# Second expert by Strassen's seven products in 924-token rounds, with combined split weights prepared by GpSimd beside the first expert

## The chip, the cores and the metric

The kernel runs on one core of one Trainium2 chip. The metric is the device time of one execution in microseconds (us), lower is better. TensorE (PE) multiplies matrices, VectorE (DVE) and ScalarE (ACT) do elementwise work and can read PSUM, GpSimd (POOL) does elementwise work on SBUF only, SyncE (SP) issues most of the DMAs. Each engine works through its own list in order and waits on semaphores.

## The reference

Three stages run one after the other on 4608 tokens (8 batches of 576), in float32:

```
p_packed = sm_attn(p, k, v)              # 32 packed keys per head
out      = sm_attn(q, p_packed, p_packed)
x        = out as (4608, 512)
xn = x / rms(x) * rms_g                  # first expert, d_ff 1536
x  = (silu(xn @ w_gate) * (xn @ w_val)) @ w_out
h  = x @ w_in                            # second expert, d_ff 2048
g  = max(h, 0) + alpha * min(h, 0)
y  = g @ w_out2
```

## The kernel before

Every large product is made from split operands: a float32 value is cast to a rounded part `hi` (float32r) and the remainder `lo`, and `three_passes` (lines 736 to 740) multiplies w_hi by hi, w_lo by hi and w_hi by lo into one PSUM bank. So each tile product is three matmuls, and each activation tile needs a cast (ScalarE) and a subtraction (VectorE) before it can be used.

The first part of the program (about 0 to 737 us) joins attention and first expert. It runs by batch. Tile b of the first expert is 24 half blocks: SiLU on ScalarE (line 1305), the product with `val` on VectorE (line 1655), the cast of h to `h_hi` (line 1313), the subtraction for `h_lo` (line 1659), and the products of two blocks earlier. Between the half blocks stands the attention of the next batch, placed by tables (`PE_PLACES`, `LATER` and the like), and the folding of the packed values into the gate and val weights (`m_hi`, `m_lo`, line 934), which reads `gv_sb`, all 12 chunks of the gate and val weights, held in SBUF. GpSimd only scales `pp_t` (line 655) and normalises `a2` (line 660) there. SyncE issues the DMAs in program order: for each half block pair the last 64 tokens of the batch go to `rest_mid` (line 531), and ScalarE waits for that store before it reuses the slot of `act_sb`. From batch 7 on SyncE also loads the second expert's weights, and GpSimd splits them (lines 711 and 713). A last tile of the gathered 8 x 64 tokens closes the first expert.

The second expert (737 us to the end) runs over nine tiles of 512 tokens. All its split weights lie in SBUF (`w2_hi_*`, `w2_lo_*`). GpSimd splits each tile's input (lines 718 and 720, four chunks of 512 columns), two tiles deep. Per tile there are 16 hidden blocks: 4 products up, 4 products down, three blocks behind. VectorE makes the leaky ReLU in two instructions (lines 1692 and 1695), ScalarE casts (line 1346), VectorE subtracts (line 1699). The down products accumulate over all 16 blocks in four PSUM banks, which ScalarE copies out (line 1355) and stores.

## Time and profile before

| | us |
|---|---|
| median of 3 runs | 1525.37 (1524.71 to 1525.61) |
| span of the profiled execution | 1524.0 |
| second expert, from its first matmul to the end of the span | 737.1 to 1524.0 |
| PE busy | 1513.6 |
| DVE busy | 726.7 |
| ACT busy | 444.7 |
| POOL busy | 193.0 |

The profiled execution's own time is known by its span alone, 1524.0 us from first to last instruction. Matmuls are pipelined, so a row's duration is longer than the distance to the next matmul: it is the distance between starts that fills the time. An instruction's recorded time contains what it waits for after it has started.

### The profile page before, as it was taken

How to read it: one execution, taken by the hardware profiler on the slowest of the kernel's cores; microseconds unless marked ns; L12 is line 12 of the kernel's file. 1: busy time of each engine (PE TensorE's matmuls, PEld its weight loads, DVE VectorE, ACT ScalarE, POOL GpSimd, SP SyncE). 2: the span in 40 equal slices, each digit the busy share in tenths (PEclk: the TensorE clock that was granted, in tenths of full speed). 3: DMA queues.
4: the chain of work that ended last, by engine and by line, in shares of the span. 5: the costliest groups of instructions: out<-in, count | busy, mean ns of one | idle time of the engine just before them, and what ended most of it. 6: DMA issues, size and time to landing. Idle time of an engine off the chain costs nothing.

```text
span 1524.0 us, 23354 instructions
## 1 busy us (share of the span) xinstructions
PE 1513.6 (99%) x9430; PEld 1258.5 (83%) x9430; DVE 726.7 (48%) x1234; ACT 444.7 (29%) x789; POOL 193.0 (13%) x197
## 2 busy tenths in 40 slices
PE   8999999999999999999999999999999999999999
PEld 5988888888888888898888888888888888888887
DVE  6674756555564746543443333333333333333333
ACT  4554544534544544422111111111111111111111
POOL 2700000000000000263342020020202001020000
PEclk9999999999999999999999999999999999999999
DMA  9313232130313230242301000010100000010000
GB/s 359 114 42 100 67 99 68 66 101 33 103 36 99 67 98 6 75 136 107 138 1 55 0 28 28 10 47 0 56 0 35 22 28 28 0 55 1 28 0 28
DMA packets 62080, 90.16 MB, mean 59 GB/s; under 512 B 17056, under 2 KB 32416, under 8 KB 61600
## 3 DMA queue, kind: packets, MB, share of 16 engines
q1 hardware_dynamic: 56944, 79.78, 16.5%
q10 hardware_dynamic: 5040, 8.98, 1.5%
q8 instruction: 75, 1.23, 0.3%
q14 instruction: 21, 0.17, 0.0%
HBM read 63.19 MB, written 25.56 MB: 58 GB/s over the span
## 4 chain that ended last, share of the span: by engine, by line
PE 98%; DVE 1%; ACT 0%; DMA 0%; issue 0%; SPq 0%; POOL 0%; POOLq 0%; DVEq 0%
PE psum L738 31%; PE psum L740 30%; PE psum L739 30%; PE psum L934 3%; PE psum L761 1%; PE psum L837 1%; PE psum L810 1%; PE psum L1074 0%; PE psum L866 0%; PE psum L865 0%; PE psum L869 0%; DMA a_keys<-a_mid 0%; PE psum L795 0%; SPq L515 0%; DMA a_mid<-a_rows 0%
## 5 line engine op out<-in xcount | busy, mean ns | idle before, releaser
L1699 DVE TENSOR_TENSOR h_lo<-g,h_hi 128x512 fp32r<-128x512 f32 x144 | 106.5, 739 | 470.2 <-ACT h_hi L1346 470.2
L1346 ACT CAST h_hi<-g 128x512 fp32r<-128x512 f32 x144 | 89.4, 621 | 632.7 <-PE psum L740 599.8
L738 PE MATMUL psum<-an_hi,m_hi 128*128 128x288 f32 x768 | 232.1, 302 | 1.2 <-DVE an_lo L1554 1.2
L740 PE MATMUL psum<-an_lo,m_hi 128*128 128x288 f32 x768 | 225.8, 294 | 0.0
L739 PE MATMUL psum<-an_hi,m_lo 128*128 128x288 f32 x768 | 225.8, 294 | 0.0
L738 PE MATMUL psum<-h_hi,ow_hi 128*128 128x512 f32 (+2 forms) x480 | 182.8, 381 | 0.0
L740 PE MATMUL psum<-h_lo,ow_hi 128*128 128x512 f32 (+2 forms) x480 | 177.7, 370 | 0.0
L739 PE MATMUL psum<-h_hi,ow_lo 128*128 128x512 f32 (+2 forms) x480 | 177.4, 370 | 0.0
L738 PEld LDWEIGHTS psum<-an_hi,m_hi 128*128 128x128 f32 x768 | 144.0, 188 | 24.1 <-issue 14.8
L1655 DVE TENSOR_TENSOR act_sb<-act_sb,psum 128x288 f32<-128x288 f32 x168 | 75.7, 451 | 154.2 <-PE psum L740 136.5
L739 PEld LDWEIGHTS psum<-an_hi,m_lo 128*128 128x128 f32 x768 | 144.3, 188 | 4.2
L740 PEld LDWEIGHTS psum<-an_lo,m_hi 128*128 128x128 f32 x768 | 144.2, 188 | 0.0
L738 PE MATMUL psum<-h_hi,w_hi_front 128*128 128x512 f32 x360 | 140.1, 389 | 0.0
L740 PE MATMUL psum<-h_lo,w_hi_front 128*128 128x512 f32 x360 | 140.1, 389 | 0.0
L740 PE MATMUL psum<-xs,w_hi_front 128*128 128x512 f32 x360 | 140.0, 389 | 0.0
L738 PE MATMUL psum<-xs,w_hi_front 128*128 128x512 f32 x360 | 140.0, 389 | 0.0
L739 PE MATMUL psum<-xs,w_lo_front 128*128 128x512 f32 x360 | 140.0, 389 | 0.0
L739 PE MATMUL psum<-h_hi,w_lo_front 128*128 128x512 f32 x360 | 140.0, 389 | 0.0
L1305 ACT ACTIVATE act_sb<-psum 128x288 f32<-128x288 f32 x168 | 69.0, 411 | 200.7 <-PE psum L740 200.1
L738 PEld LDWEIGHTS psum<-h_hi,ow_hi 128*128 128x128 f32 x480 | 90.2, 188 | 38.2 <-issue 27.3
L1692 DVE TENSOR_SCALAR act_sb<-psum,alpha_sb 128x512 f32<-128x512 f32 x144 | 107.4, 746 | 2.0 <-PE psum L740 2.0
L740 PEld LDWEIGHTS psum<-h_lo,ow_hi 128*128 128x128 f32 x480 | 90.3, 188 | 16.3
(183 smaller groups left out, 2405.6 us busy)
## 6 DMA issues: line engine op xcount, KB each, us to landing
k_sb<-k_t SPq DMA_DIRECT2D x16, 576.0 KB, 5.2
q_sb<-q_t SPq DMA_DIRECT2D x8, 1152.0 KB, 5.5
xs_raw<-y_mid SPq DMA_DIRECT2D x9, 1024.0 KB, 5.2
out_t<-o_sb ACTq DMA_DIRECT2D x34, 256.0 KB, 2.0
gv_sb<-w_gv SPq DMA_DIRECT2D x6, 1024.0 KB, 17.1
...
a_keys<-a_mid SPq DMA_DIRECT2D x24, 160.0 KB, 3.3
```

The costliest lines, as they stand in the source:

```text
L738: nc.tensor.matmul(dst, w_hi, hi, start=start, stop=False)
L739: nc.tensor.matmul(dst, w_lo, hi, start=False, stop=False)
L740: return nc.tensor.matmul(dst, w_hi, lo, start=False, stop=stop)
L761: mm = nc.tensor.matmul(dst, p_sb[dims, pair, :], k_sb[dims, pair, h * HALF:(h + 1) * HALF], start=True, stop=True)
L810: mm = nc.tensor.matmul(pp_ps(c, e)[PACK * pair:PACK * (pair + 1), :], a_keys[:, e * PAIRS + pair, j, :], v_sb[:, j, head * HEAD_DIM:(head ...
L837: mm = nc.tensor.matmul(s2_ps(e)[PACK * pair:PACK * (pair + 1), :], pp_t[dims, pair, :], q[dims, pair, h * HALF:(h + 1) * HALF], start=Tru ...
L934: mm = nc.tensor.matmul(psum[keys, m_bank(c, j) + e, :].rearrange("p (f n) -> p f n", f=2), pp_tg[dims, pair, :], gv_sb[dims, 2 * j:2 * j ...
L1305: nc.scalar.activation(act_sb[:, s, half * HALF:(half + 1) * HALF], gate_ps, ACT.Silu).then_inc(silu_done, 1)
L1346: nc.scalar.copy(h2_hi[:, f % 2, :], g32[:, f % 2, :]).then_inc(g_hi_done, 1)
L1655: nc.vector.tensor_tensor(dst, dst, val_ps, ALU.mult).then_inc(h32_done, 1)
L1692: nc.vector.tensor_scalar(act2_sb[:, s, :], h, 0.0, alpha_sb[:, f:f + 1], ALU.min, ALU.mult).then_inc(neg_done, 1)
L1699: nc.vector.tensor_tensor(h2_lo[:, s, :], g32[:, s, :], h2_hi[:, s, :].bitcast(F32), ALU.subtract).then_inc(g_lo_done, 1)
```

## The change

The second expert is computed by Strassen's scheme in Winograd's form. Both its products are cut into two by two blocks: for the up product two halves of the 512 model dimensions, two neighbouring hidden blocks (a duo, 8 of them), and two halves of a round's tokens; for the down product the same with the roles exchanged. Instead of eight block products there are seven, of sums and differences of blocks. A round has 924 tokens (2 x 462; the last 2 x 456), and there are five rounds. The matmuls are 462 columns wide.

- Weights: GpSimd (`combine`) makes from each of 32 parts of raw weights four combinations, casts the seven matrices to hi and subtracts for lo. This stands in the first expert's tiles 1 to 7, up to two parts before `scaled` and three behind it. SyncE stores hi and lo to DRAM (`w_up`, `w_down`), in runs of 512 bytes, and later streams them back page by page (30 pages a round, of 786 KB or 1 MB) into a ring of four slots.
- To make room, the first expert holds only 6 chunks of `gv_sb` and loads each pair of chunks again in every batch (33 loads of 1 MB).
- Input: GpSimd makes four differences of 2 x 462 columns and splits seven matrices of 2 x 462 columns a round, as soon as the previous round's up products are done; two sums of outputs stand between the fourth and the fifth split.
- Up: 42 matmuls a duo. VectorE and ScalarE evict seven PSUM results (three of them accumulate onto an evicted bank), ScalarE makes the two halves of the leaky ReLU, VectorE joins them.
- Down: 56 units a round, each one staged block times two output halves, 6 matmuls. ScalarE casts the block to `stage_hi`, VectorE subtracts for `stage_lo`; four stages. VectorE makes the differences of blocks (`difference`) and sums of outputs (`down_sums`) in between, by a table of places (`BESIDE_UNITS`). All down products of a round follow all its up products.

The instruction counts in the second expert: 3456 matmuls of 512 columns before, 5 x 672 = 3360 of 462 (456) now.

```diff
+PRODUCTS = 7
...
+PART_PLACES = {b: ([5 * (b - 1), 5 * (b - 1) + 1], [5 * (b - 1) + n for n in range(2, 5)]) for b in range(1, BATCH)}
...
+WIDTHS = [462, 462, 462, 462, 456]
...
+UNIT_SLOTS, STAGES = 4, 4
...
+    w_up = nc.dram_tensor("w_up", (DUOS, P, PRODUCTS, 2, 2, P), F32, kind="Internal").ap()
+    w_down = nc.dram_tensor("w_down", (PRODUCTS, P, DUOS, 2, 2, P), F32, kind="Internal").ap()
...
+            def load_part(n):
+                slot = n % PART_SLOTS
+                reached(sp, part_out[slot], 32 * (n // PART_SLOTS))
+                raw = parts_raw[slot]
+                sp.dma_start(raw[:, 0:PRODUCTS:3, :], w2_parts[n, :, 0:3, :]).then_inc(part_in[slot], 16)
+                sp.dma_start(raw[:, 4, :], w2_parts[n, :, 3, :]).then_inc(part_in[slot], 16)
+
+            def store_part(n):
+                sp.wait_ge(part_ready, n + 1)
+                slot, j, side = n % PART_SLOTS, n % (2 * DUOS) // 2, n % 2
+                for level, src in ((0, parts_hi[slot]), (1, parts_lo[slot])):
+                    if n < 2 * DUOS:
+                        dst = w_up[j, :, :, side, level, :]
+                    else:
+                        dst = w_down[:, :, j, side, level, :].rearrange("i p n -> p i n")
+                    sp.dma_start(dst, src[:].bitcast(F32)).then_inc(part_out[slot], 16)
...
+            def move_parts(b, f):
...
+                    for n in range(PART_SLOTS):
+                        load_part(n)
+                if f == 3:
+                    for n in early:
+                        store_part(n)
+                if f == 4:
+                    for n in early:
+                        if n + PART_SLOTS < PARTS:
+                            load_part(n + PART_SLOTS)
...
+            def load_x(t):
+                w, at = WIDTHS[t], STARTS[t]
+                for slot, rows, cols in ((0, 0, 0), (2, 0, 1), (4, 2, 0), (5, 2, 1)):
+                    sp.dma_start(x_raw[:, slot, :, 0:w],
+                                 y_mid[:, rows:rows + 2, at + cols * w:at + (cols + 1) * w]).then_inc(x_in, 16)
...
+            def load_page(t, n):
+                q, slot = PAGES * t + n, (PAGES * t + n) % UNIT_SLOTS
...
+                if q >= UNIT_SLOTS:
+                    free_t, free_n = (q - UNIT_SLOTS) // PAGES, (q - UNIT_SLOTS) % PAGES
+                    if free_n < 2 * DUOS:
+                        sp.wait_ge(up_mm, PRODUCTS * (DUOS * free_t + free_n // 2) + UP_PARTS[free_n % 2][1])
+                    else:
+                        sp.wait_ge(unit_mm, UNITS * free_t + DUOS * (free_n // 2 - DUOS) + DOWN_PARTS[free_n % 2][1])
+                sp.dma_start(ring[:, slot, 0:stop - first_unit].bitcast(F32), src).then_inc(ring_in[slot], 16)
+
...
+            def combine(n):
...
+                nc.gpsimd.tensor_tensor(raw[:, 2, :], raw[:, 3, :], raw[:, 6, :], ALU.add).then_inc(part_step, 1)
+                pool.wait_ge(part_step, done + 1)
+                nc.gpsimd.tensor_tensor(raw[:, 3, :], raw[:, 0, :], raw[:, 3, :], ALU.subtract).then_inc(part_step, 1)
+                nc.gpsimd.tensor_tensor(raw[:, 1, :], raw[:, 2, :], raw[:, 0, :], ALU.subtract).then_inc(part_step, 1)
+                pool.wait_ge(part_step, done + 3)
+                nc.gpsimd.tensor_tensor(raw[:, 5, :], raw[:, 4, :], raw[:, 1, :], ALU.subtract).then_inc(part_step, 1)
+                pool.wait_ge(part_step, done + 4)
+                nc.gpsimd.tensor_copy(hi[:], raw[:]).then_inc(part_step, 1)
+                pool.wait_ge(part_step, done + 5)
+                nc.gpsimd.tensor_tensor(lo[:], raw[:], hi[:].bitcast(F32), ALU.subtract).then_inc(part_ready, 1)
...
+                early, late = PART_PLACES.get(c - 1, ([], []))
+                for n in early:
+                    combine(n)
+                if c < BATCH:
+                    scaled(c)
+                for n in late:
+                    combine(n)
+                if c < BATCH:
+                    normed(c, 0)
+                    normed(c, 1)
...
+            def differences(t):
+                w, done = WIDTHS[t], X_STEPS * t
+                pool.wait_ge(x_in, 16 * 4 * (t + 1))
+                for n, (to, of, less) in enumerate(((3, 5, 2), (2, 2, 0), (1, 5, 2), (6, 4, 1))):
+                    nc.gpsimd.tensor_tensor(x_raw[:, to, :, 0:w], x_raw[:, of, :, 0:w], x_raw[:, less, :, 0:w],
+                                            ALU.subtract).then_inc(x_step, 1)
+                    pool.wait_ge(x_step, done + n + 1)
+
+            def split_x(t, i):
+                w, done = WIDTHS[t], X_STEPS * t + 4 + i
+                nc.gpsimd.tensor_copy(x_hi[:, i, :, 0:w], x_raw[:, i, :, 0:w]).then_inc(x_step, 1)
+                pool.wait_ge(x_step, done + 1)
+                nc.gpsimd.tensor_tensor(x_lo[:, i, :, 0:w], x_raw[:, i, :, 0:w], x_hi[:, i, :, 0:w].bitcast(F32),
+                                        ALU.subtract).then_inc(x_ready, 1)
...
+            def sums_of_outs(t):
...
+                nc.gpsimd.tensor_tensor(out_f[:, :, 0:w], out_e[:, :, 0:w], out_h[:, :, 0:w], ALU.add).then_inc(f_done, 1)
+                pool.wait_ge(f_done, t + 1)
+                nc.gpsimd.tensor_tensor(out_h[:, :, 0:w], out_r[:, :, 0:w], out_h[:, :, 0:w], ALU.add).then_inc(q_done, 1)
...
+            differences(0)
+            for i in range(PRODUCTS):
+                split_x(0, i)
+            for t in range(ROUNDS):
+                if t + 1 < ROUNDS:
+                    differences(t + 1)
+                    for i in range(4):
+                        split_x(t + 1, i)
+                sums_of_outs(t)
+                if t + 1 < ROUNDS:
+                    for i in range(4, PRODUCTS):
...
+            def up(t, j):
+
+                w, n = WIDTHS[t], DUOS * t + j
+                freed = {0: (c11_copied, n), 1: (u_done, n), 2: (c12_done, n), 3: (c21_done, n),
+                         4: (p1_copied, n + 1), 5: (c22_part, n + 1), 6: (c22_done, n + 1)}
+                for part, (begin, end) in enumerate(UP_PARTS):
...
+                    for i in range(begin, end):
...
+                        dst = four_ps(UP_BANKS[i], w)
+                        for k in range(2):
+                            mm = three_passes(dst, weights[:, i - begin, k, 0, :], weights[:, i - begin, k, 1, :],
+                                              x_hi[:, i, k, 0:w], x_lo[:, i, k, 0:w], k == 0 and i < 4, k == 1, i >= 4)
...
+            def down2(t, p):
...
+                        u = UNITS * t + DUOS * p + j
+                        pe.wait_ge(stage_lo_done, u + 1)
+                        for side in range(2):
...
+            def stage_hi_of(t, u):
+                w, p, j, n = WIDTHS[t], u // DUOS, u % DUOS, UNITS * t + u
+                i = DOWN_ORDER[p]
...
+                reached(act, unit_mm, n - STAGES + 1)
+                nc.scalar.copy(stage_hi[:, n % STAGES, 0:w], raw_of(i, j, w)).then_inc(stage_hi_done, 1)
...
+            def negative(t, j, f):
...
+                nc.scalar.activation(below[:, f, :, 0:w], g_sb2[:, j, f, :, 0:w], ACT.Relu, scale=-1.0).then_inc(below_done, 1)
...
+            def up_sums(t, j, name):
+                w, n = WIDTHS[t], DUOS * t + j
+                u, c22 = shared[:, n % 2, 0:w], g_sb2[:, j, 1, 1, 0:w]
+                if name == "u":
+                    dve.wait_ge(up_mm, PRODUCTS * n + 2)
+                    dve.wait_ge(p1_copied, n + 1)
+                    nc.vector.tensor_tensor(u, first_p[:, 0:w], four_ps(1, w), ALU.add).then_inc(u_done, 1)
...
+            def joined(t, j, f):
+                w, n = WIDTHS[t], DUOS * t + j
+                dve.wait_ge(above_done, 2 * n + f + 1)
+                both = g_sb2[:, j, f, :, 0:w]
+                nc.vector.scalar_tensor_tensor(out=both, in0=below[:, f, :, 0:w], scalar=minus_alpha[:, 2 * j + f:2 * j + f + 1],
+                                               in1=both, op0=ALU.mult, op1=ALU.add).then_inc(g_done, 1)
...
+            def stage_lo_of(t, u):
+                w, p, j, n = WIDTHS[t], u // DUOS, u % DUOS, UNITS * t + u
+                dve.wait_ge(stage_hi_done, n + 1)
+                nc.vector.tensor_tensor(stage_lo[:, n % STAGES, 0:w], raw_of(DOWN_ORDER[p], j, w),
+                                        stage_hi[:, n % STAGES, 0:w].bitcast(F32), ALU.subtract).then_inc(stage_lo_done, 1)
+
+            def difference(t, two, name):
...
+                if name == "t4":
+                    dve.wait_ge(stage_lo_done, UNITS * t + 4 * DUOS + 2 * two + 2)
+                    nc.vector.tensor_tensor(changed, g_sb2[:, js, 1, 0, 0:w], changed, ALU.subtract).then_inc(t4_done, 1)
...
+            BESIDE_UNITS = {7: ["t1 0"], 9: ["t1 1"], 11: ["t1 2"], 13: ["t1 3"],
+                            18: ["t2 0"], 20: ["t2 1"], 23: ["t2 2"], 25: ["t2 3"], 28: ["e"],
+                            34: ["t4 0"], 36: ["t4 1"], 37: ["o11"], 38: ["t4 2"], 40: ["t4 3"],
+                            44: ["o22"], 45: ["e2"], 46: ["h2"], 52: ["o12"]}
```

On GpSimd in the first expert, where the weights of attention batch 2 are folded. Before (`pp_tg` is `scaled`, `a2` with `rinv` is `normed`):

```order
L698 CAST ow_hi_86<-ow_raw_88 128x512
L700 TENSOR_TENSOR ow_lo_87<-ow_raw_88,ow_hi_86 128x256
L701 TENSOR_TENSOR ow_lo_87<-ow_raw_88,ow_hi_86 128x256
L655 TENSOR_TENSOR pp_tg_78<-pp_t_77,g_sb_51 128x128
L660 TENSOR_TENSOR a2_68<-a2_68,rinv_61 128x576 x2
L655 TENSOR_TENSOR pp_tg_78<-pp_t_77,g_sb_51 128x128
```

Now (`parts_raw` and the rest are `combine`; the 128x896 rows are its cast and its subtraction):

```order
L837 TENSOR_TENSOR parts_raw1_115<-parts_raw1_115 128x128
L839 TENSOR_TENSOR parts_raw1_115<-parts_raw1_115 128x128
L840 TENSOR_TENSOR parts_raw1_115<-parts_raw1_115 128x128
L842 TENSOR_TENSOR parts_raw1_115<-parts_raw1_115 128x128
L844 CAST parts_hi1_113<-parts_raw1_115 128x896
L846 TENSOR_TENSOR parts_lo1_114<-parts_raw1_115,parts_hi1_113 128x896
L783 TENSOR_TENSOR pp_tg_79<-pp_t_78,g_sb_51 128x128
L837 TENSOR_TENSOR parts_raw2_118<-parts_raw2_118 128x128
L839 TENSOR_TENSOR parts_raw2_118<-parts_raw2_118 128x128
L840 TENSOR_TENSOR parts_raw2_118<-parts_raw2_118 128x128
L842 TENSOR_TENSOR parts_raw2_118<-parts_raw2_118 128x128
L844 CAST parts_hi2_116<-parts_raw2_118 128x896
```

One part ends and another begins around `scaled`; both are new there.

On GpSimd in the second expert. Before (the splitting of a tile's input, and of the weights that come last):

```order
L718 CAST xs<-xs_raw 128x512
L720 TENSOR_TENSOR xs<-xs_raw,xs 128x512
L718 CAST xs<-xs_raw 128x512
L720 TENSOR_TENSOR xs<-xs_raw,xs 128x512
L711 CAST w_hi_mid<-w_raw_mid 128x1024
L713 TENSOR_TENSOR w_lo_mid<-w_raw_mid,w_hi_mid 128x1024
```

Now (`x_hi` and `x_lo` split the input, `out_f` and `out_h` are the two sums of outputs):

```order
L872 CAST x_hi<-x_raw 128x2x462
L874 TENSOR_TENSOR x_lo<-x_raw,x_hi 128x2x462
L872 CAST x_hi<-x_raw 128x2x462
L874 TENSOR_TENSOR x_lo<-x_raw,x_hi 128x2x462
L883 TENSOR_TENSOR out_f<-out_e,out_h 128x924
L885 TENSOR_TENSOR out_h<-out_r,out_h 128x924
L872 CAST x_hi<-x_raw 128x2x462
L874 TENSOR_TENSOR x_lo<-x_raw,x_hi 128x2x462
```

The sums stand behind four of the seven splits of the next round's input.

On VectorE in the second expert, in the down products. Before (a whole hidden block is three rows):

```order
L1641 COPY y_last<-psum 128x512 x2
L1687 UNCONDITIONAL_BRANCH
L1687 ISA
L1692 TENSOR_SCALAR act_sb<-psum,alpha_sb 128x512
L1695 SCALAR_TENSOR_TENSOR g_124<-psum,act_sb 128x512
L1699 TENSOR_TENSOR h_lo<-g_124,h_hi 128x512
L1691 REGISTER_ALU
L1692 TENSOR_SCALAR act_sb<-psum,alpha_sb 128x512
L1695 SCALAR_TENSOR_TENSOR g_124<-psum,act_sb 128x512
```

Now (`g_sb` from `g_sb` are the differences, `out_e` and `out_r` the sums of outputs):

```order
L1950 TENSOR_TENSOR stage_lo<-g_sb_124,stage_hi 128x462 x2
L1961 TENSOR_TENSOR g_sb_124<-g_sb_124 128x2x462
L1950 TENSOR_TENSOR stage_lo<-g_sb_124,stage_hi 128x462 x3
L1974 TENSOR_TENSOR out_e<-out_r,psum 128x924
L1950 TENSOR_TENSOR stage_lo<-g_sb_124,stage_hi 128x462 x6
L1964 TENSOR_TENSOR g_sb_124<-g_sb_124 128x2x462
L1950 TENSOR_TENSOR stage_lo<-g_sb_124,stage_hi 128x462 x2
L1964 TENSOR_TENSOR g_sb_124<-g_sb_124 128x2x462
L1950 TENSOR_TENSOR stage_lo<-g_sb_124,stage_hi 128x462
L1978 TENSOR_TENSOR out_r<-out_r,psum 128x924
L1950 TENSOR_TENSOR stage_lo<-g_sb_124,stage_hi 128x462
```

Each `stage_lo` belongs to one unit of 6 matmuls, and other work on two SBUF tensors stands between them.

## Rows read from the trace of the kernel before

**Rows 1.** The page: busy time by engine, and the chain that ended last.
```profile
PE 1513.6 (99%) x9430; PEld 1258.5 (83%) x9430; DVE 726.7 (48%) x1234; ACT 444.7 (29%) x789; POOL 193.0 (13%) x197
...
PE 98%; DVE 1%; ACT 0%; DMA 0%; issue 0%; SPq 0%; POOL 0%; POOLq 0%; DVEq 0%
```

**Rows 2.** Line 738 asked alone: duration min/median/max ns, first and last start.
```profile
L738 PE MATMUL psum<-xs,w_hi_front x360: 389/389/389, 737.1 to 1476.3; 128*128 128x512 f32 x180
...
L738 PE MATMUL psum<-h_hi,w_hi_back x72: 389/389/389, 824.1 to 1519.8; 128*128 128x512 f32 x72
```

**Rows 3.** TensorE timeline in the first expert: start us, us, instruction.
```profile
664.70 0.29 PE L738 MATMUL psum<-an_hi,m_hi 128*128 128x288 f32 x1
...
666.15 0.30 PE L740 MATMUL psum<-an_lo,m_hi 128*128 128x288 f32 x1
```

**Rows 4.** Groups of instructions in the second expert on VectorE and ScalarE.
```profile
L1699 DVE TENSOR_TENSOR h_lo<-g,h_hi 128x512 fp32r<-128x512 f32 x144 | 106.5, 739 | 470.2 <-ACT h_hi L1346 470.2
L1695 DVE SCALAR_TENSOR_TENSOR g<-psum,act_sb 128x512 f32<-128x512 f32 x144 | 99.6, 692 | 4.9
L1346 ACT CAST h_hi<-g 128x512 fp32r<-128x512 f32 x144 | 89.4, 621 | 632.7 <-PE psum L740 599.8 <-DVE g L1695 25.8 <-ACT o_sb L1355 7.1
L1355 ACT COPY o_sb<-psum 128x512 f32<-128x512 f32 x32 | 18.8, 589 | 37.8 <-PE psum L740 27.1 <-ACT o_sb L1355 10.7
```

**Rows 5.** GpSimd timeline as the first expert ends and the second begins.
```profile
669.76 2.40 POOL L713 TENSOR_TENSOR w_lo_front<-w_raw_front,w_hi_front 128x1024 fp32r<-128x1024 f32 x1
...
707.64 0.61 POOL L718 CAST xs<-xs_raw 128x512 fp32r<-128x512 f32 x1
...
710.59 1.29 POOL L720 TENSOR_TENSOR xs<-xs_raw,xs 128x512 fp32r<-128x512 f32 x1
711.83 1.07 POOL L718 CAST xs<-xs_raw 128x512 fp32r<-128x512 f32 x1
...
750.30 1.04 POOL L711 CAST w_hi_mid<-w_raw_mid 128x1024 fp32r<-128x1024 f32 x1 [36.02 <-DMA w_raw_mid<-w]
751.42 2.40 POOL L713 TENSOR_TENSOR w_lo_mid<-w_raw_mid,w_hi_mid 128x1024 fp32r<-128x1024 f32 x1
```

**Rows 6.** VectorE timeline over the same stretches.
```profile
670.66 2.04 DVE L1659 TENSOR_TENSOR h_lo<-act_sb,h_hi 128x512 fp32r<-128x512 f32 x1 [0.69 <-ACT h_hi L1313]
672.63 0.44 DVE L1655 TENSOR_TENSOR act_sb<-act_sb,psum 128x288 f32<-128x288 f32 x1
...
710.61 1.82 DVE L1668 TENSOR_TENSOR h_lo<-rest,h_hi 128x512 fp32r<-128x512 f32 x1 [1.81 <-ACT h_hi L1323]
...
751.61 2.75 DVE L1699 TENSOR_TENSOR h_lo<-g,h_hi 128x512 fp32r<-128x512 f32 x1 [4.53 <-ACT h_hi L1346]
```

**Rows 7.** The val product of line 1655 (one SBUF and one PSUM input) over the span.
```profile
L1655 DVE TENSOR_TENSOR act_sb<-act_sb,psum x168: 394/455/456, 121.8 to 699.1; 128x288 f32<-128x288 f32 x168
```

**Rows 8.** Engines by stretch: busy us (x instructions), PE clock, DMA share, GB/s.
```profile
18.00:24.00 6.00, 4.27 (x25) 2.52 (x30) 5.56 (x13) 1.43 (x3) 1.16 (x1) 1.00 1.02 409
...
20.00:48.00 28.00, 25.30 (x234) 18.68 (x235) 22.41 (x43) 17.75 (x33) 16.81 (x23) 1.00 1.00 362
...
328.00:404.00 76.00, 76.00 (x616) 63.35 (x615) 43.40 (x83) 36.82 (x68) 3.23 (x3) 1.00 0.30 84
...
632.00:700.00 68.00, 68.00 (x429) 61.47 (x427) 27.46 (x38) 17.84 (x38) 35.51 (x20) 1.00 0.38 129
```

**Rows 9.** GpSimd timeline inside one tile of the first expert.
```profile
401.83 0.40 POOL L655 TENSOR_TENSOR pp_tg<-pp_t,g_sb 128x128 f32<-128x128 f32 x1 [37.34 <-ACT pp_t L1161]
446.88 2.83 POOL L660 TENSOR_TENSOR a<-a,rinv 128x576 f32<-128x576 f32 x2 [44.64 <-DVE rinv L1534]
```

**Rows 10.** VectorE timeline at the end of one tile of the first expert.
```profile
456.77 0.75 DVE L1549 TENSOR_TENSOR an_lo<-a,an_hi 128x576 fp32r<-128x576 f32 x1
457.54 0.69 DVE L1659 TENSOR_TENSOR h_lo<-act_sb,h_hi 128x512 fp32r<-128x512 f32 x1
```

**Rows 11.** DMA issues: KB each, median us to landing.
```profile
xs_raw<-y_mid SPq DMA_DIRECT2D x9, 1024.0 KB, 5.2
out_t<-o_sb ACTq DMA_DIRECT2D x34, 256.0 KB, 2.0
...
a_keys<-a_mid SPq DMA_DIRECT2D x24, 160.0 KB, 3.3
```

590 lines of the change are left out of this document (376 added, 214 removed).

## Prediction

> **What bounds the kernel now.** I read the page first: PE is busy 99% of the span and the chain that ended last is PE for 98% [rows 1]. Then I asked for the matmuls of one line, for the distance between starts. In the second expert the first matmul starts at 737.1 us, and the last first-pass matmul, the 3454th of 3456, at 1519.8 us [rows 2]: 782.7 / 3453 = 0.2267 us for 512 columns. In the first expert twelve matmuls of 288 columns take eleven distances from 664.70 to 666.15 us [rows 3], 0.1318 us each. So the second expert is a row of matmuls with no gap, 3456 x 0.2267 = 783.5 us. Next come the groups of VectorE and ScalarE there: each idles for hundreds of us, waiting for PE or for the other [rows 4]. Last I laid the timelines of GpSimd and VectorE side by side [rows 5, 6], because the change gives much new work to both.
>
> What these show matters most. GpSimd's subtraction of 710.59 us ends at 711.88. VectorE's `h_lo` started at 710.61 and takes 1.82 us, though a free one takes 0.69 (the time of line 1695 [rows 4]): it ends 0.55 us behind GpSimd's, which is 512 columns at the 1.06 ns a column that lies between the durations of lines 1655 (0.455 at 288 [rows 7]) and 1695 (0.692 at 512 [rows 4]). GpSimd's next cast in turn takes 1.07 us where a free one takes 0.61. At 751.61 `h_lo` takes 2.75 us behind a subtraction that ends at 753.82. So an instruction of VectorE with two SBUF inputs and one of GpSimd exclude each other for their whole length and take turns, one each. The val product of line 1655, with one input in PSUM, took at most 456 ns in 168 runs [rows 7]: it is exempt. The Trainium skill, GPSIMD Engine Reference, Key points, says that GpSimd shares its SBUF interfaces with VectorE and contends with instructions in a two-port mode or with two SBUF inputs; the trace agrees, and shows the price, which that section does not give.
>
> **Matmuls.** A line through the two distances has 0.424 ns per column. So 462 columns take 0.2267 - 50 x 0.000424 = 0.2055 us, 456 take 0.2029. Four rounds of 672 at 0.2055 are 552.4 us, one at 0.2029 is 136.3: 688.7. That removes 94.8 us. If the distance went with columns alone it would be 0.2046 (3 us less); the upper bound is the rate of 512 columns, 0.2267, with 71 us more, and nothing speaks for that.
>
> **Up phase.** A duo is 42 matmuls, 8.63 us. VectorE has five sums from PSUM, two joinings of 924 columns and one difference. By those two lines one takes 0.64 at 462 and 1.12 at 924. That is 6 x 0.64 + 2 x 1.12 = 6.1 us. ScalarE has two copies (0.589 at 512) and four Relu of 924 columns, bounded by 0.6 below and 1.2 (two of 512) above: at most 6 us. The bank of product 5 is wanted 6.2 us into a duo and free near 4.5, that of product 6 at 7.4 and free near 6.3. GpSimd rests in this phase. I take no cost; if I am wrong by the 1 us of that slack it is 40 us over 40 duos.
>
> **Down phase without GpSimd.** A unit of 6 matmuls is 1.233 us. VectorE's list for 56 units: 56 subtractions, 12 differences and 7 sums of 924 columns. From start to start these take some 0.08 less than their durations: 56 x 0.56 + 19 x 1.04 = 51 us of 69. ScalarE: 56 x 0.6 plus two copies, 36 us. A stage is freed three units (3.7 us) before it is needed and cast plus subtraction take 1.3 us. This alone would cost nothing; I take 1 us in all for the joins between phases.
>
> **Down phase with GpSimd.** This is the term that decides. For the next round GpSimd runs 4 differences, 7 casts and 7 subtractions, and 2 sums of outputs, all of 924 columns, beginning when the previous up products are done. Its durations, between 1.29 (512) and 2.40 (1024) for two inputs, 0.61 and 1.04 for casts [rows 5]: 2.19 and 0.97 at 924. In the contested case above the interface changes hands some 0.14 us before the recorded end, so it is held for 2.05 and 0.83: 13 x 2.05 + 7 x 0.83 = 32.5 us. These are 20 instructions, and in the turn taking VectorE gets one two-SBUF instruction between each two: 56 of 68 are `stage_lo` (462 x 1.06 ns = 0.49 us), 12 are differences (0.98), mean 0.576. So the stretch lasts 32.5 + 20 x 0.576 = 44.0 us, and in it VectorE prepares 20 x 56/68 = 16.5 units, 20.3 us of PE. PE waits 23.7 us a round. Four rounds prepare a next one: 95 us. The fifth has two sums only, inside the slack. Lower bound: 0, were all these waits inside the slack, as in the kernel before, where GpSimd works on 8 instructions per 87 us tile. Upper bound: if hands change only at recorded ends, 20 x 0.28 more a round, 117 us in all. I take 95, since its two constants come from contested rows. What is queued behind a waiting `stage_lo` is VectorE's whole list; PE waits for it, and ScalarE's cast waits for PE to free the stage.
>
> **GpSimd in the first expert.** Each of 32 parts is four sums of 128 columns (0.40 each, by `pp_tg` [rows 9]), a cast and a subtraction of 896 (0.93, 2.13), about 5 us with gaps. Three late parts run after `scaled` at 401.8 and two early ones after `normed` at 446.9, which has 45 us of idling before it [rows 9], so GpSimd's own deadlines hold. VectorE pays. Near 650 to 700 us the same kind of work (35.5 of 68 us busy) hid: PE lost nothing [rows 8], and a `h_lo` of 2.04 us at 670.66 only made the val product of 672.63 start without idling [rows 6]. But there VectorE had 27.5 us of work in 68; in a full tile it has 43.4 in 76 [rows 8]. And at a tile's end an_lo, `h_lo` and an_lo stand in a row [rows 10] while the down products of that tile wait for this `h_lo`. Bounds: 0 by the first stretch, 32 x 2.13 = 68 us if every long subtraction stalled PE in full. I take 0.4 us a part, 12 us, near the lower row: the blocks alternate and most waits fall in slack.
>
> **DMA.** Now 33 loads of 1 MB, 64 stores of 448 KB in 512-byte runs and the raw parts are added to tiles of 85 us that move 84 GB/s [rows 8]: 6 + 4.6 + 1.3 MB a tile, 140 GB/s more, 224 in all. Read alone the queues reach 362 [rows 8]. The pages are 29.4 MB in some 160 us, 184 GB/s, and are asked for about 12 us ahead; 1 MB lands in 5.2 us [rows 11]. No cost there. Three parts stored at once (2.75 MB) delay the small stores behind them for which ScalarE waits: 8 to 14 us against some 11 of slack, so 0 to 3 us a tile, 0 to 18 in six. I take 2.
>
> **Tail.** The last output sum is of 924 columns and its store 473 KB instead of 256 KB (2.0 us [rows 11]): 1 us more.
>
> **Sum.** 1524.0 - 94.8 + 1 + 95 + 12 + 2 + 1 = 1540.2 us of span. The runs lie 1.4 us above the span (1525.37 median): 1542 us.
>
> **Rivals.** *PE stays the bound* (0.08). The turn taking costs nothing, the rest as above: 1542 - 95 = 1447, and with VectorE less disturbed in the first expert too, 1437. For it: GpSimd's splitting beside the second expert never stopped PE before. Against it: it had 8 instructions per tile then, and now 20 within 69 us of work that needs a two-SBUF instruction every 1.0 us. *Milder turns* (0.13). VectorE has the next instruction ready and gets two between GpSimd's: the stretch is 32.5 + 40 x 0.576 = 55.5 us with 33 units, 40.6 us; PE waits 14.9 a round, 60 in all: 1507. No row shows two in a row while GpSimd waits. *The slower side: everything collides* (0.19). The first expert decides: at 1.5 us a part and 3 us a tile for the queue it costs 48 + 18 instead of 14, so 1594; or half of that with the upper bound of the turns, 1590. I put 1580 on it. It decides from the point where VectorE's delay in a tile exceeds the 1 to 1.5 us between its val product and PE's next use of the bank.
>
> *The clock.* PE now works in pieces of 1.2 us with gaps of 1.4 for 44 us a round. At 18 to 24 us PE was busy 4.27 of 6 us and the granted clock stayed 1.00 [rows 8], its 2.4 GHz level. Were it to fall to 1.2 GHz, a unit would take 2.5 us against VectorE's 2.67 per unit in the stretch, so only one or two units behind each of eight stretches would show: 10 to 20 us, part of the third rival. The Trainium skill, TensorE: Matmul & The Clock Gate, Part 1, says that the array falls to half rate when it has been idle; no row here shows a fall.
>
> **Chances.** The forecast 0.57, with its own range 1515 to 1570; the rivals 0.08, 0.13, 0.19; 0.03 beyond. Below about 1522 us are the first two rivals and a tenth of the forecast: 0.27 for faster by over 0.2%. The runs of before spread by 0.06%, so 0.2% (3 us) is about what can be told apart. Within it 0.06, slower 0.67. The range 1492 to 1594 holds the forecast, the milder turns and most of the slower side.
>
> **What would show it.** Right, if in the down phases of rounds 1 to 4 `stage_lo` takes near 2.5 us where GpSimd is busy and 0.64 elsewhere, PE's wait on it comes near 95 us, rounds 1 to 4 take about 161 us and the fifth 137. The matmul distance should be 0.205. Wrong, if the mean of `stage_lo` stays under 1 us, if PE waits in the up phase, or if the first expert ends far from 750 us.

## Result: 1560.0 us, 2.3% slower, and the profile after

The changed kernel takes 1560.0 us (median of 4 runs, 1558.6 to 1563.0), the kernel before 1525.3 us in the same comparison: ratio 1.023, 95% interval 1.0218 to 1.0243. The forecast was 1542. The sign and the range held; the change of 35 us is twice the 17 us forecast.

The page of the changed kernel answers [rows 1]: busy time, three rows of the slices (the granted clock among them), and the chain that ended last.
```profile
span 1558.7 us, 23935 instructions
...
PE 1478.5 (95%) x9334; PEld 1254.2 (80%) x9334; DVE 1070.6 (69%) x1496; ACT 691.7 (44%) x1141; POOL 444.3 (29%) x379
...
PE   8999999999999999999998799979997899789998
...
POOL 2704224343313234325003700181007300640000
PEclk9999999999999999999999899989999999989999
...
PE 79%; DVE 17%; ACT 2%; DMA 1%; issue 1%; SPq 0%; POOL 0%; ACTq 0%; DVEq 0%; POOLq 0%
```
PE was 98% of the chain and is 79%; VectorE has the other 17%. The slices dip four times in the second expert, where GpSimd's row fills.

One line of matmuls and two groups answer [rows 2, 4].
```profile
L904 PE MATMUL psum<-x_hi,ring x560: 365/373/382, 757.1 to 1482.8; 128*128 128x462 f32 x150, 128*128 128x456 f32 x37
```
```profile
L904 PE MATMUL psum<-stage_hi,ring 128*128 128x462 f32 (+1 forms) x560 | 222.9, 398 | 54.6 <-DVE stage_lo L1950 54.4
L1950 DVE TENSOR_TENSOR stage_lo<-g_sb,stage_hi 128x462 fp32r<-128x462 f32 (+1 forms) x240 | 245.6, 1052 | 29.5 <-ACT stage_hi L1531 28.6
...
L904 PE MATMUL psum<-h_hi,ow_hi 128*128 128x512 f32 (+2 forms) x480 | 183.5, 382 | 10.4 <-DVE h_lo L1883 10.4
```
The second expert begins at 757.1 us (737.1 before). Its rounds begin at 757.1, 920.2, 1084.6, 1247.6 and 1413.2, so they take 163 to 166 us, and the last one 141. Their up phases are 71.1 us each (70.2 in the fifth), their down phases 92.0, 93.3, 91.8, 94.6 and 70.9: the same matmuls, 21 to 24 us longer wherever a next round is prepared. The page books only 54.4 us of that as PE's wait on `stage_lo`: a gap is counted from a matmul's recorded end, which lies behind the next one's usual start, and part of the rest is matmuls at a lower clock (see *Sum* further down).

The timelines of GpSimd and VectorE in round 1's down phase (start us, us, instruction, idling before it) answer [rows 5, 6].
```profile
844.72 9.92 POOL L866 TENSOR_TENSOR x_raw<-x_raw 128x924 f32<-128x924 f32 x4 [119.75 <-DMA x_raw<-y_mid]
854.71 1.73 POOL L872 CAST x_hi<-x_raw 128x924 fp32r<-128x924 f32 x1
856.52 2.43 POOL L874 TENSOR_TENSOR x_lo<-x_raw,x_hi 128x924 fp32r<-128x924 f32 x1
...
876.17 2.53 POOL L883 TENSOR_TENSOR out_f<-out_e,out_h 128x924 f32<-128x924 f32 x1 [4.83 <-DVE out_e L1974]
```
```profile
845.61 7.00 DVE L1950 TENSOR_TENSOR stage_lo<-g_sb,stage_hi 128x462 fp32r<-128x462 f32 x3 [0.62 <-ACT stage_hi L1531]
852.53 3.09 DVE L1961 TENSOR_TENSOR g_sb<-g_sb 128x924 f32<-128x924 f32 x1
855.54 3.90 DVE L1950 TENSOR_TENSOR stage_lo<-g_sb,stage_hi 128x462 fp32r<-128x462 f32 x2
```
Three `stage_lo` take 7.0 us and four differences of GpSimd 9.9 us: near 2.4 us each, one of the one engine behind one of the other, as forecast. The trace, instruction by instruction, says the same for all four rounds: wherever two GpSimd instructions follow each other without a pause (72 pairs), exactly one of VectorE's two-SBUF instructions ends between their ends.

### The profile page after: what moved, and what is told of

Its sections match the earlier page's. It is cut to its first block, busy times and chain, and to the rows that moved or that the text cites. A ratio compares the mean times of both kernels' runs of the same rounds, so it can differ in the third digit from the quotient of the medians.

```text
span 1558.7 us, 23935 instructions
## 1 busy us (share of the span) xinstructions
PE 1478.5 (95%) x9334; PEld 1254.2 (80%) x9334; DVE 1070.6 (69%) x1496; ACT 691.7 (44%) x1141; POOL 444.3 (29%) x379
## 4 chain that ended last, share of the span: by engine, by line
PE 79%; DVE 17%; ACT 2%; DMA 1%; issue 1%; SPq 0%; POOL 0%; ACTq 0%; DVEq 0%; POOLq 0%
PE psum L904 25%; PE psum L906 24%; PE psum L905 24%; DVE stage_lo L1950 9%; PE psum L1102 3%; DVE g_sb L1961 2%; DVE e L1672 1%; DVE h_lo L1883 1%; DVE g_sb L1964 1%; DMA rest_mid<-act_sb 1%; PE psum L927 1%; DVE max L1668 1%; DVE an_lo L1773 1%; PE psum L976 0%; DVE act_sb L1879 0%
## 5 line engine op out<-in xcount | busy, mean ns | idle before, releaser
L904 PE MATMUL psum<-stage_hi,ring 128*128 128x462 f32 (+1 forms) x560 | 222.9, 398 | 54.6 <-DVE stage_lo L1950 54.4
L1950 DVE TENSOR_TENSOR stage_lo<-g_sb,stage_hi 128x462 fp32r<-128x462 f32 (+1 forms) x240 | 245.6, 1052 | 29.5 <-ACT stage_hi L1531 28.6
L1531 ACT CAST stage_hi<-g_sb 128x462 fp32r<-128x462 f32 (+1 forms) x240 | 138.8, 578 | 238.8 <-PE psum L906 238.6
L906 PE MATMUL psum<-stage_lo,ring 128*128 128x462 f32 (+1 forms) x560 | 217.3, 388 | 0.0
L905 PE MATMUL psum<-stage_hi,ring 128*128 128x462 f32 (+1 forms) x560 | 216.8, 387 | 0.0
L904 PE MATMUL psum<-x_hi,ring 128*128 128x462 f32 (+1 forms) x560 | 209.7, 374 | 0.0
L906 PE MATMUL psum<-x_lo,ring 128*128 128x462 f32 (+1 forms) x560 | 209.0, 373 | 0.0
L905 PE MATMUL psum<-x_hi,ring 128*128 128x462 f32 (+1 forms) x560 | 208.1, 372 | 0.0
L904 PE MATMUL psum<-h_hi,ow_hi 128*128 128x512 f32 (+2 forms) x480 | 183.5, 382 | 10.4 <-DVE h_lo L1883 10.4
L866 POOL TENSOR_TENSOR x_raw<-x_raw 128x924 f32<-128x924 f32 (+1 forms) x20 | 49.1, 2457 | 501.3 <-DMA x_raw<-y_mid 500.1
L904 PEld LDWEIGHTS psum<-stage_hi,ring 128*128 128x128 f32 x560 | 110.8, 198 | 87.9 <-DVE stage_lo L1950 57.1
```

Source lines behind the costliest of these rows:

```text
L866: nc.gpsimd.tensor_tensor(x_raw[:, to, :, 0:w], x_raw[:, of, :, 0:w], x_raw[:, less, :, 0:w], ALU.subtract).then_inc(x_step, 1)
L904: nc.tensor.matmul(dst, w_hi, hi, start=start, stop=False, skip_group_check=onto)
L905: nc.tensor.matmul(dst, w_lo, hi, start=False, stop=False, skip_group_check=onto)
L906: return nc.tensor.matmul(dst, w_hi, lo, start=False, stop=stop, skip_group_check=onto)
L1531: nc.scalar.copy(stage_hi[:, n % STAGES, 0:w], raw_of(i, j, w)).then_inc(stage_hi_done, 1)
L1950: nc.vector.tensor_tensor(stage_lo[:, n % STAGES, 0:w], raw_of(DOWN_ORDER[p], j, w), stage_hi[:, n % STAGES, 0:w].bitcast(F32), ALU.subtra ...
```

## Experiments

The theory (T1): a VectorE instruction with two SBUF inputs and one of GpSimd exclude each other and take turns, and PE waits for the VectorE instruction. The rival (T2): the new DMA traffic (301 MB in all, mean 193 GB/s) delays PE or VectorE. Apart from both stands the matmul distance (from the start of one to the start of the next), which was 0.2117 us at 462 columns where 0.2055 was forecast. Times are medians beside 1525.3 to 1525.7 of the kernel before.

**1. GpSimd's x work on 2 columns.** Differences, splits and the x loads of rounds 2 to 5 lose all but 2 columns.
```diff
-                w, done = WIDTHS[t], X_STEPS * t
+                w, done = WIDTHS[t] if t == 0 else 2, X_STEPS * t
```


> Edit: from the second round on, GpSimd's differences, casts and subtractions of x, and the x loads, work on 2 columns instead of 462 (the outputs of rounds 2 to 5 are then not the reference's). The pages' traffic stays as it is (29.4 of 37 MB a round). Theory 1 (two-SBUF instructions of VectorE and instructions of GpSimd take turns, and PE waits for VectorE's stage_lo): the stretches of turns go; only the two output sums of 924 columns are left. Each of rounds 1 to 4 loses its 21 us of PE waits: 1560 - 4 x 21 = 1476 us, between 1470 and 1482; round distance 142 to 143 us; PE's wait on stage_lo under 8 us. Theory 2 (the traffic of pages, in the queues or at the memory, delays VectorE's and PE's reads): 80% of that traffic is unchanged, so at most a fifth of the waits goes: 1543 us or more.

Measured 1472.0 us (1467.3 to 1474.6), 88 less than the changed kernel. Rounds took 142, 141, 143, 143 us. The groups of PE and VectorE:
```profile
L904 PE MATMUL psum<-stage_hi,ring 128*128 128x462 f32 (+1 forms) x560 | 208.0, 371 | 2.4 <-DVE stage_lo L1950 2.4
...
L1950 DVE TENSOR_TENSOR stage_lo<-g_sb,stage_hi 128x462 fp32r<-128x462 f32 (+1 forms) x240 | 166.5, 710 | 47.5 <-ACT stage_hi L1531 46.7
```
PE's wait on `stage_lo` went from 54.4 to 2.4 us, with pages at full traffic: this is what T1 expects. GpSimd still issued as many instructions, only very short ones. So their number alone costs little; what costs is how long each one holds up the VectorE instruction behind it.

**2. Pages of a quarter.** From the second round on a page load moves one unit.
```diff
+                if t > 0:
+                    sp.dma_start(ring[:, slot, 0:1].bitcast(F32), src[:, 0:1]).then_inc(ring_in[slot], 16)
```


> Edit: from the second round on each page load moves one unit's quarter of the page (the other weights in the slot stay from an earlier page, so the outputs of those rounds are not the reference's). GpSimd's and VectorE's work is unchanged; DMA moves about 7.5 MB of pages a round instead of 29.4. Theory 1 (turns): no change, 1560 us within 3; stage_lo of 462 columns still has a mean of 1.1 us over all and PE's round distance is 163 to 165 us. Theory 2 (traffic): rounds 2 to 4 lose most of their waits of PE, and the fifth too: 1560 - 3 x 16 = 1512 us or less. If the matmul distance of 0.2117 us at 462 columns comes from traffic, it falls to 0.2055 here from round 2 on, 4 x 4 us less.

Measured 1559.4 us (1557.4 to 1560.5). Round 2's down phase (991 to 1084 us), first of the changed kernel, then of this one: busy us (x instructions) of PE, weight loads, VectorE, ScalarE, GpSimd, then clock, DMA share, GB/s.
```profile
991.00:1084.00 93.00, 81.18 (x337) 67.70 (x336) 83.54 (x76) 34.98 (x58) 42.75 (x20) 0.89 0.56 190
```
```profile
991.00:1084.00 93.00, 79.15 (x343) 65.86 (x342) 84.01 (x77) 35.00 (x58) 44.59 (x20) 0.94 0.22 71
```
190 GB/s became 71; VectorE and GpSimd were about as busy as before, and PE about as idle. All up phases of 462 columns took 71.1 us as before. T2 is out for the second expert, and page traffic is out as the cause of the matmul distance.

**3. GpSimd in quarters.** Its two-input instructions (not the casts) become four each.
```diff
+                for k, at, end, last in pieces(w):
+                    op = nc.gpsimd.tensor_tensor(x_lo[:, i, k, at:end], x_raw[:, i, k, at:end],
+                                                 x_hi[:, i, k, at:end].bitcast(F32), ALU.subtract)
```


> Edit: GpSimd's four differences, seven subtractions and two output sums a round are each issued as four instructions of a quarter of the elements (231 columns of one k); the casts stay whole. Same results, same traffic, same elements. Theory 1 (turns, one VectorE instruction between each two of GpSimd's): 52 short and 7 long instructions instead of 20; VectorE gets 59 turns in a stretch of about 32.5 + 1 + 59 x 0.576 = 67.5 us instead of 20 in 44, so PE waits 7 to 14 us a round instead of 21: 1505 to 1532 us, and stage_lo beside GpSimd takes about 1.1 us (0.55 behind a quarter of 0.55) where it took 2.5. Theory 2 (traffic): no change, 1560. A third reading, that what counts is GpSimd's busy time and not the number of turns: no change or a little slower, 1560 to 1570, for the fixed cost of 39 more instructions a round.

Measured 1537.9 us (1536.4 to 1539.0): 22 less, with more GpSimd work (519 us busy instead of 444). This was short of the turn arithmetic, and one of VectorE's waits in the second expert shows why: us in total, times, longest.
```profile
DVE out_r L1990 <- POOL out_h L896: 35.4, 4, 9.3
```
GpSimd's stretch is longer now, and it comes to its output sums 9 us a round after VectorE could have used them.

**4. Quarters, sums behind the second split.** GpSimd's two output sums move forward in its own order.
```diff
-                    for i in range(4):
+                    for i in range(2):
                         split_x(t + 1, i)
                 sums_of_outs(t)
```


> Edit: the quarters, and GpSimd's two output sums now stand behind its second split of the next round instead of behind the fourth. In the run of the quarters VectorE's first sum of out_r waits 9.3 us a round for GpSimd's sum of out_h, and PE 10 us for the stage_lo behind it: the new wait that the longer stretch brought. VectorE has out_e ready at 863.8 us and wants the sum at 876.4; behind the second split GpSimd would do both sums from 870.5 to 875.6. Theory 1 (turns, and this wait as what was left of the gain): 1538 - 4 x 9 = 1502 us, between 1497 and 1510, faster than the kernel before. Rival: the elements decide, and PE falls behind by the same amount elsewhere in the stretch, where it now waits 0.3 to 0.9 us at a time: 1530 us or more.

Measured 1513.0 us (1512.8 to 1514.9), 25 less, ratio 0.992 (0.991 to 0.994) to the kernel before; 11 us above the 1502 expected, since a wait of some 3 us a round was left in the same place (3.1 us idle before PE's start of 881.6 us). With it the kernel is faster than before by less than 1%, but clear of the noise.

**5. The ladder of widths.** Behind the last matmul of the kernel before, 36 matmuls at each of 14 widths.
```diff
+            for wide in (512, 510, 508, 504, 496, 480, 464, 462, 456, 448, 384, 320, 288, 256):
+                for n in range(12):
+                    cols = slice(P * (n % 4), P * (n % 4) + P)
+                    three_passes(psum[:, n % 4, 0:wide], hi[:, cols], lo[:, cols], ..., True, True)
```


> The kernel before, with a ladder behind its last matmul: for 512, 510, 508, 504, 496, 480, 464, 462, 456, 448, 384, 320, 288 and 256 columns, 36 matmuls each (12 products in three passes) with no wait between them, to the same banks. It measures the distance from matmul to matmul by width, with nothing else running. Theory a (512 columns alone run at the low price): every width from 256 to 510 has 0.458 ns a column, 0.2336 at 510. Theory b (a width that is a multiple of 16 is cheap): 464, 480 and 496 come at 0.2059, 0.2129, 0.2198. Theory c (the distance at 462 was set by the traffic or by the loads of weights in after; the run with small pages speaks against it, its up products being as far apart as before): here 462 comes at 0.2055. The added time is about 36 x 14 x 0.17 = 90 us, so 1610 us in all.

First and last matmul of two widths, 35 distances apart:
```profile
1569.52 0.37 PE L738 MATMUL psum<-xs,w_hi_front 128*128 128x464 f32 x1
...
1576.83 0.37 PE L740 MATMUL psum<-xs,w_hi_front 128*128 128x464 f32 x1
1577.04 0.37 PE L738 MATMUL psum<-xs,w_hi_front 128*128 128x462 f32 x1
...
1584.45 0.38 PE L740 MATMUL psum<-xs,w_hi_front 128*128 128x462 f32 x1
```
So 464 columns take 0.2089 us and 462 take 0.2117: the narrower one costs more. The others, each good to 0.0003: 510 0.2269, 508 0.2277, 504 0.2271, 496 0.2234, 480 0.2169, 456 0.2083, 448 0.2026, 384 0.1743, 320 0.1466, 288 0.1320, 256 0.1197. None of the three theories had it. 510 isn't dear (against a). 464 is cheaper than 462, by 0.003 and not by 0.007 us, but 504 and 508, which are no multiples of 16, cost a column as little as 496 does (0.451, 0.448 and 0.450 ns; 462 costs 0.458), so b isn't shown as a rule either. And c is dead: 462 columns take 0.2117 with nothing else running. Why 462 and 456 are dear stays open.

**6. Combining on 2 columns** (first expert; the stores stay).
```diff
+                some = slice(0, P if n < PART_SLOTS else 2)
```


> Edit: for parts 4 to 32 GpSimd's sums, cast and subtraction of w2's parts, and the raw loads, work on 2 columns instead of 128 (the second expert's weights are then wrong); the stores of 448 KB each stay. The second expert's first matmul starts at 737.1 us before and at 757.1 after. Theory 1 (turns with the combining delay h_lo and an_lo, and PE waits for them): it starts at 738 to 742 us here, and the tile's-end h_lo of 2.5 us are 0.7 to 1.8. Theory 2 (the traffic of the parts, of which 4.6 of 5.9 MB a tile are stores): 752 us or more. The second expert itself is unchanged, 798 to 801 us.

**7. Few stores** (first expert; the combining stays).
```diff
+                    few = slice(0, PRODUCTS if n < 2 * PART_SLOTS else 1)
+                    sp.dma_start(dst[:, few], src[:, few].bitcast(F32)).then_inc(part_out[slot], 16)
```


> Edit: from the seventh part on each store moves one of seven products (64 KB instead of 448), and the pages are read from the three duos that are stored whole (the second expert's weights are then wrong); GpSimd's combining and the raw loads stay. Theory 1 (turns): the second expert's first matmul starts at 755 to 757 us as in after; what could go is the wait of 4 us in the last tile, where a store of rest_mid lands late, if the part stores made it late rather than the loads of x and of pages. Theory 2 (store traffic): 742 us or less. The second expert is unchanged, 798 to 801 us.

One run each, 1542.3 and 1551.8 us. The second expert's first matmul in 6, then in 7:
```profile
L905 PE MATMUL psum<-x_hi,ring x560: 364/374/383, 738.3 to 1464.6; 128*128 128x462 f32 x150, 128*128 128x456 f32 x37
```
```profile
L905 PE MATMUL psum<-x_hi,ring x560: 362/373/382, 748.5 to 1474.0; 128*128 128x462 f32 x150, 128*128 128x456 f32 x37
```
Without the combining all but 1 us of the 20 is back (T1). But fewer stores also gave 9 us, and PE's wait on `h_lo` fell from 10.4 to 2.4 us, which T1 had not expected. (Kernels with the same first expert began the second one between 751.2 and 757.1 us, so 3 to 9 us can be put down to the stores.) At one tile's end, in the changed kernel and then in 7:
```profile
465.46 0.47 POOL L837 TENSOR_TENSOR parts_raw<-parts_raw 128x128 f32<-128x128 f32 x1 [4.39 <-DMA parts_raw<-w_parts]
...
468.51 2.49 POOL L846 TENSOR_TENSOR parts_lo<-parts_raw,parts_hi 128x896 fp32r<-128x896 f32 x1
...
468.96 2.59 DVE L1883 TENSOR_TENSOR h_lo<-act_sb,h_hi 128x512 fp32r<-128x512 f32 x1
```
```profile
457.88 0.58 POOL L838 TENSOR_TENSOR parts_raw<-parts_raw 128x128 f32<-128x128 f32 x1 [0.83 <-DMA parts_raw<-w_parts]
...
461.02 2.12 POOL L847 TENSOR_TENSOR parts_lo<-parts_raw,parts_hi 128x896 fp32r<-128x896 f32 x1
...
465.05 0.95 DVE L1884 TENSOR_TENSOR h_lo<-act_sb,h_hi 128x512 fp32r<-128x512 f32 x1
```
The raw part is loaded behind the stores, in SyncE's order. With full stores it lands 4.4 us after GpSimd is free, which puts the long subtraction onto the tile's last `h_lo` (2.59 us, 0.69 when free [rows 10]). With few it runs before. The changed kernel shows this at six tile ends: the raw part comes 3.8 to 4.8 us late, and PE then waits 1.4 to 1.9 us for `h_lo`. In experiment 7 it shows at the first of them alone, where the stores are still whole. The turns are the price; the traffic set where it is paid.

**8. Sums behind the first split, and the parts' subtraction in four pieces,** on experiment 4's version.
```diff
+                for at in range(0, PRODUCTS, 2):
+                    few = slice(at, min(at + 2, PRODUCTS))
+                    op = nc.gpsimd.tensor_tensor(lo[:, few], raw[:, few], hi[:, few].bitcast(F32), ALU.subtract)
```


> Edit, on the version with quarters: GpSimd's output sums stand behind its first split instead of its second, and its subtraction for the parts of w2 in the first expert is issued as four instructions of at most two products (256 columns) instead of one of 896. Theory 1 (turns decide in both experts): PE's one wait of 3.2 us a round, in front of VectorE's sum of out_r, goes (4 x 3.2 = 13 us); in the first expert h_lo at a tile's end waits for a piece of 0.63 us and not for 2.1, so PE's waits on h_lo fall from 9.0 us to under 3 and the second expert's first matmul comes at 746 to 750 instead of 755.2. 1513 - 13 - 7 = 1493 us, between 1488 and 1501. Rival: the stretch of turns only shifts, and the 3.2 us come back as shorter waits; and the traffic of the parts, not GpSimd's instructions, delays h_lo: 1508 us or more.

Measured 1485.9 us (1484.6 to 1486.9), 27 less than experiment 4: better than expected. The down phases fell from 82 to 79 us each, and the second expert began at 740.3 instead of 755.2 us:
```profile
L919 PE MATMUL psum<-x_hi,ring x560: 365/373/382, 740.3 to 1408.9; 128*128 128x462 f32 x150, 128*128 128x456 f32 x37
```
So some 15 us of the first expert's 20 (11 to 17 by the spread of its starts) hung on 32 instructions of 2.25 us, though in pieces they are busy longer (102 us instead of 72). The raw parts come as late as before, but PE then waits at most 0.7 us.

**9. Widths 464 and 448** on that version, and **10. the same on the changed kernel.**
```diff
-WIDTHS = [462, 462, 462, 462, 456]
+WIDTHS = [464, 464, 464, 464, 448]
```


> Edit, on the version with the sums behind the first split: token widths 464, 464, 464, 464, 448 instead of 462 x 4 and 456. The ladder gave 0.2089 us at 464 and 0.2026 at 448, against 0.2117 at 462 and 0.2083 at 456. 672 matmuls a round: 672 x (4 x 0.0028 + 0.0057) = 11 us less, were PE the bound throughout; in the down phases VectorE sets the pace in the stretches of turns (near 60 of 82 us), so there the shorter distance gives little: 5 to 11 us less than that version. Rival: the distance of this kernel doesn't follow the ladder, no change within 2 us.

> Edit, on the changed kernel itself: widths 464, 464, 464, 464, 448 instead of 462 x 4 and 456, nothing else. By the ladder 672 x (4 x 0.0028 + 0.0057) = 11.4 us less of matmuls; in the 44 us a round in which VectorE and GpSimd take turns VectorE sets the pace, so PE keeps about 0.75 of it: 1560 - 8.5 = 1551.5 us, between 1548 and 1554. Rival: in this kernel the distance isn't what the ladder shows (traffic, the ring's weights), and 464 columns take what 462 take: 1560, or 2 us more, for the two extra columns of VectorE's and GpSimd's work.

Measured 1478.6 us (1477.6 to 1479.4), 7.3 less than experiment 8, and 1548.6 us (1546.9 to 1555.0), 11.4 less than the changed kernel. In the up phases the distance is near the ladder's: 0.2089 or 0.2100 us at 464 columns, 0.2026 at 448. In the down phases of the changed kernel it gives little, as expected: those of 464 columns took 93.3, 93.3, 93.3 and 92.7 us. The profiled execution was the slowest of the five, at 1555.0 us; what brought the others 5 to 8 us lower no profile shows, but their granted clock was 0.980 to 0.985 where this one's was 0.975.

**11. Widths 512 and 256**, with three slots in the ring.
```diff
-WIDTHS = [462, 462, 462, 462, 456]
+WIDTHS = [512, 512, 512, 512, 256]
...
-UNIT_SLOTS, STAGES = 4, 4
+UNIT_SLOTS, STAGES = 3, 4
```


> Edit, on the version with the sums behind the first split: token widths 512, 512, 512, 512, 256, and three slots in the ring of pages instead of four (the memory has no room for the fourth). The ladder and the runs gave 0.2267 us at 512 and 0.1197 at 256: 672 x (4 x 0.2267 + 0.1197) = 689.8 us against 709.1, 19 us less; and the fourth round prepares only 256 columns for the last one, so its stretch of turns is half as long, and most of the 7 us that PE waits there goes. So 20 to 26 us less than that version. Rival: three slots hold pages for 3.4 to 5.4 us less, and the last round's units of 0.72 us are under VectorE's 0.65 us each with no slack: PE waits for pages or for stage_lo, and it is within 5 us of that version, or slower.

Measured 1481.9 us (1478.0 to 1485.1): 4 less than experiment 8, not 20. PE's waits in the second expert:
```profile
PE psum L919 <- DVE stage_lo L1965: 20.5, 28, 1.3
PE psum L919 <- DMA ring<-w_up: 6.8, 5, 2.0
PE psum L919 <- DMA ring<-w_down: 3.5, 3, 1.7
```
10 us are now waits for pages, and the wait for VectorE is the 21 us it was. In rounds 1 to 4 the distance follows the ladder (up phases of 76.2 us), and the fourth round waits for VectorE under 1 us, as expected. The loss is in the fifth: all the waits for pages stand there, and it takes 97.5 us where 672 distances of 0.1197 are 80.4. Its matmuls are half as wide and want the same pages in about half the time (315 GB/s in its up phase). Whether a fourth slot would have covered that was not tested, since slots and widths were changed together.

**12. x casts on ScalarE**, on experiment 9's version.
```diff
+                    if t + 1 < ROUNDS and u in X_CASTS:
...
+                        nc.scalar.copy(x_hi[:, i, :, 0:w], x_raw[:, i, :, 0:w]).then_inc(x_cast, 1)
```


> Edit, on the version with widths 464 and 448: in rounds 1 to 4 the seven casts of 928 columns for the next round move from GpSimd to ScalarE, which is busy 46% there, spread over units 19 to 41. Each cast held VectorE's interface for some 0.85 us and was longer than the 0.55 of a quarter: seven of GpSimd's 59 turns go, 6 us of holding and 7 turns a round. PE waits some 8 us a round in the stretch. Theory 1 (turns): 3 to 6 us a round less, 1478.6 - 4 x 4 = 1463 us, between 1455 and 1470, with GpSimd's stretch some 9 us shorter. Rival: a ScalarE cast of about 1 us makes the stage_hi behind it late, PE falls to the last staged unit and waits for ScalarE instead: 1475 to 1485.

Measured 1473.6 us (1472.0 to 1474.3), 5 less, ratio 0.966 (0.964 to 0.967) to the kernel before: right in direction, a third in size, and neither theory's range held it. GpSimd's stretch ends at 882.3 instead of 889.1 us, but PE's waits stood before 878 already, so most of what was freed lay where VectorE had caught up. This is the fastest version, 52 us under the kernel before.

## Where the forecast was wrong in size, and what in it was right

The forecast had the direction and the mechanism, but its 17 us are half of the 35 measured. The terms for the matmuls and for the first expert were 20.7 and 6 us too small, the one for the down phases 8 us too large.

*Matmuls: mis-sized, the largest error.* The step that failed is "462 columns take 0.2267 - 50 x 0.000424 = 0.2055 us", a line through two widths. 462 take 0.2117 and 456 0.2089 here (up phases of 71.1 and 70.2 us, by 336), so 709.4 us instead of 688.7: 20.7 us. The ladder shows that no line goes through these points; 0.2117 x 288 / 462 = 0.1320 is the value at 288, while 512 is cheap. The forecast's own row of 288 columns, taken as a rate a column, would have given 0.1318 x 462 / 288 = 0.2114. It tried that scaling from 512 alone. Its upper end, every matmul at 0.2267, was said to have nothing for it; the truth lay 0.3 of the way there (and 3360 x 0.2267 is 73 us more, not 71).

*Up phase at no cost: right.* No wait of PE there.

*Down phase and turns: right, 96 forecast, 88 measured.* The down phases are longer than their matmuls by 20.9, 22.2, 20.7 and 23.5 us, and by 0.7 in the fifth. GpSimd's two stretches in round 1 are 844.7 to 871.3 and 876.2 to 893.2, 43.6 us; forecast 44.0. With the true distance the same arithmetic gives 44.0 - 16.5 x 1.27 = 23.0 a round. Experiments 1 to 4 show the cause: page traffic doesn't matter (2); what matters is how long GpSimd holds VectorE up at each turn. With as many GpSimd instructions, but of 4 elements each, the waits went (1), and with the same elements in shorter instructions half of them went (3 and 4). In round 1, 16 `stage_lo` and 4 differences take turns with GpSimd's 20 instructions, and 16.5 and 3.5 were forecast. Of the 16, ten take 2.5 to 2.6 us, behind a two-input instruction, and five 1.4 us, behind a cast; the "near 2.5" left the casts out. The mean is 1.05 us over the whole run.

One sign did not come: PE's wait on `stage_lo` "near 95 us" is 54.4 us in the rows. From start to start the waits are 63 us, and 25 us are matmuls at the lower clock (*Sum*, below).

*GpSimd in the first expert with the DMA: 14 forecast, 20.0 measured.* The price was right in kind and not in place. The working spread 0.4 us over each part; in truth PE waited 10.4 us in seven waits on `h_lo`, at tile ends, and 3.4 us in five on the val product. The forecast had named the tile's end and gave it no price of its own. The 2 us for the queue came as one wait, of ScalarE for a late store of rest_mid in the last tile:
```profile
ACT act_sb L1488 <- DMA rest_mid<-act_sb: 4.0, 1, 4.0
```
But the stores did more by shifting GpSimd onto the tile's end (experiment 7), which the forecast, with a term for each apart, could not have.

*Tail: +1 forecast;* from the last first-pass start to the end of the span it was 4.2 us [rows 2] and is 5.0:
```profile
L904 PE MATMUL psum<-stage_hi,ring x560: 363/373/753, 828.2 to 1553.7; 128*128 128x462 f32 x150, 128*128 128x456 f32 x37
```

*Sum.* 1540.2 + 20.7 - 8 + 6 = 1558.9 us of span, against 1558.7. Of the rivals, milder turns did not come. The third rival's place in the first expert, the val product, had the smaller part of the waits, and its price was three times too high. Its clock part came true, at less cost than its 10 to 20 us. Stretches of the changed kernel, columns as above:
```profile
856.00:860.00 4.00, 2.90 (x7) 2.07 (x8) 4.00 (x3) 0.44 (x1) 3.92 (x3) 0.65 0.00 0
860.00:864.00 4.00, 1.80 (x7) 1.25 (x7) 4.00 (x3) 0.71 (x2) 3.92 (x3) 0.92 0.77 260
864.00:868.00 4.00, 4.00 (x13) 3.47 (x13) 4.00 (x3) 0.58 (x1) 3.92 (x3) 0.57 0.01 2
```
The granted clock, 1.00 at its 2.4 GHz level, is 0.65 and 0.57 in the first and the third of these, so for part of them it is at the 1.2 GHz level; there matmuls start 0.385 us apart instead of 0.212. Before the two falls PE was busy 1.52 us of 852 to 856 and 1.80 of 860 to 864. VectorE sets the pace, so a slow matmul mostly hides: the ones from 857.3 us on are followed by another wait of 2.2 us. They show only behind the last long wait of a stretch, which in rounds 2 and 4 is some 1.4 us each. By the recorded starts and ends this is 3 us in all, an estimate; no run changed the clock alone. In experiment 8, where PE waits at most 1.3 us at a time and is busy 3.06 and 2.90 us of 862 to 866 and 866 to 870, the clock stayed at 1.00. The longest wait alone doesn't tell: in round 2 of the changed kernel the clock fell at 1017.7 us behind waits of 0.7, 0.9 and 1.0 us (PE busy 2.08 us of 1014 to 1018).
